# Seven block products for w_in as well, in pair sets, and block sums by adding transfers

## The reference

```python
h = x @ w_in;  r = np.maximum(h, 0.0);  g = r * r;  x = g @ w_out      # first MLP
h = x @ w_in;  g = h * (1.0 / (1.0 + np.exp(-h)));  out = g @ w_out     # second MLP
```

## Time and profile before

| | before |
|---|---|
| median of 3 runs | 532.4 us (532.11 to 532.63) |
| profiled execution | 531.69 us, span 529.9 us |
| granted TensorE clock, mean | 0.999 |
| PE busy | 521.0 us (98%), 2628 instructions |
| DVE busy | 350.9 us (66%) |
| ACT busy | 260.3 us (49%) |
| POOL busy | 77.5 us (15%), all before 95 us |
| DMA | 42.17 MB |

### The profile page before, as it was taken

The page is one execution under the profiler, slowest core; times in us unless marked ns, Lnnn a source line. Parts: engine busy times, 40 slices in busy tenths (PEclk is TensorE's granted clock), DMA queues, the critical chain, the costliest instruction groups (busy, mean ns, idle before and its releaser), DMA issues.

```text
span 529.9 us, 7052 instructions
## 1 busy us (share of the span) xinstructions
PE 521.0 (98%) x2628; PEld 440.0 (83%) x2628; DVE 350.9 (66%) x604; ACT 260.3 (49%) x404; POOL 77.5 (15%) x52
## 2 busy tenths in 40 slices
PE   7999999999999999999999999999999999999996
PEld 5333335799999999999999999999999999999996
DVE  3487878797687533667799746556764245568975
ACT  5999996154454333544444344454444144454220
POOL 1899999000000000000000000000000000000000
PEclk9999999999999999999999999999999999999999
DMA  7798611051302202522032025202211241020447
GB/s 222 196 241 227 180 41 33 28 141 59 80 0 80 59 1 59 141 59 67 13 80 61 1 61 139 61 18 62 60 49 32 61 138 36 26 80 10 102 74 106
DMA packets 82181, 42.17 MB, mean 80 GB/s; under 512 B 26848, under 2 KB 79072, under 8 KB 82144
## 3 DMA queue, kind: packets, MB, share of 16 engines
q1 hardware_dynamic: 77984, 40.32, 29.2%
q10 hardware_dynamic: 4128, 1.38, 1.1%
q0 software_dynamic: 32, 0.00, 0.0%
HBM read 38.93 MB, written 2.75 MB: 79 GB/s over the span
## 4 chain that ended last, share of the span: by engine, by line
PE 94%; DMA 2%; DVE 1%; ACT 1%; issue 1%; SPq 1%; ACTq 0%
PE banks L558 27%; PE banks L557 27%; PE banks L559 27%; PE banks L477 4%; PE banks L470 4%; PE banks L498 2%; PE banks L467 1%; DMA qk_raw<-in_k_dram 1%; DMA qk_raw<-in_q_dram 1%; PE banks L489 1%; ACT prob L683 1%; SPq L324 1%; ACT prob L690 0%; DVE asum L917 0%; ACTq L660 0%
## 5 line engine op out<-in xcount | busy, mean ns | idle before, releaser
L557 PE MATMUL banks<-x_hi,w_hl 128*128 128x448 f32 x384 | 139.4, 363 | 0.0
L558 PE MATMUL banks<-x_lo,w_hl 128*128 128x448 f32 x384 | 139.4, 363 | 0.0
L559 PE MATMUL banks<-x_hi,w_hl 128*128 128x448 f32 x384 | 138.3, 360 | 0.0
L558 PE MATMUL banks<-g_lo,w_hl 128*128 128x448 f32 (+1 forms) x340 | 122.7, 361 | 0.0
L557 PE MATMUL banks<-g_hi,w_hl 128*128 128x448 f32 (+1 forms) x340 | 122.5, 360 | 0.0
L559 PE MATMUL banks<-g_hi,w_hl 128*128 128x448 f32 (+1 forms) x340 | 121.7, 358 | 0.0
L557 PEld LDWEIGHTS banks<-x_hi,w_hl 128*128 128x128 f32 x384 | 72.1, 188 | 6.9 <-issue 1.4
L559 PEld LDWEIGHTS banks<-x_hi,w_hl 128*128 128x128 f32 x384 | 71.8, 187 | 5.1
L558 PEld LDWEIGHTS banks<-x_lo,w_hl 128*128 128x128 f32 x384 | 72.1, 188 | 3.8
L975 DVE TENSOR_TENSOR w_hl<-w_raw,w_hl 128x768 fp32r<-128x768 f32 x32 | 31.9, 996 | 55.4 <-ACT w_hl L716 55.2
L557 PEld LDWEIGHTS banks<-g_hi,w_hl 128*128 128x128 f32 x340 | 63.8, 188 | 4.8
(11 more groups left out here) (63 smaller groups left out, 509.8 us busy)
## 6 DMA issues: line engine op xcount, KB each, us to landing
w_raw<-in_moe_w_in_dram SPq DMA_DIRECT2D x32, 384.0 KB, 3.4
w_raw<-in_moe_w_out_dram SPq DMA_DIRECT2D x24, 512.0 KB, 5.2
qk_raw<-in_k_dram SPq DMA_DIRECT2D x44, 112.0 KB, 2.7
qk_raw<-in_q_dram SPq DMA_DIRECT2D x44, 112.0 KB, 3.3
v_t<-in_v_dram SPq DMA_DIRECT2D x24, 96.0 KB, 2.8
out_dram<-rows SPq DMA_DIRECT2D x38, 56.0 KB, 2.2
qk_raw<-in_k_dram ACTq DMA_DIRECT2D x4, 112.0 KB, 3.0
qk_raw<-in_q_dram ACTq DMA_DIRECT2D x4, 112.0 KB, 4.0
```

The source lines that it names most:

```text
L557: pe.matmul(dst, hi[:, kk, :], mov_hi, start=start, stop=False, skip_group_check=onto)
L558: pe.matmul(dst, hi[:, kk, :], mov_lo, start=False, stop=False, skip_group_check=onto)
L559: return pe.matmul(dst, lo[:, kk, :], mov_hi, start=False, stop=stop, skip_group_check=onto)
```

## The change

- w_in is computed with seven block products too, in all stages but the first. A *pair set* makes two hidden chunks by two batches: 7 products of 3 x 3 passes. x therefore needs seven operands (`x_all`, B11 to T4, high and low), of which four are sums (`xt_make`).
- A layer has three stages of 2, 3 and 3 chunk pairs instead of two of 8 chunks. The order of sets in a layer is: the stage's pair sets, then its three group sets. The very first stage has two *plain sets* (72 passes each) in place of pair sets, and x's sums are made beside them. All sets are numbered in `sets`; 0 and 1 are plain.
- Signs are arranged so that a block sum of weights is an addition. The four sums of a set (q1 to q4, one product each: 1, 4, 2, 5) are no longer made by DVE but by DMA transfers that add onto their destination, issued by GpSimd (q1 from DRAM, the others from SBUF). The blocks that are added to are loaded once more for it: six loads of one block each and four adding transfers per set.
- In a pair set ACT copies the results of products 0 to 2 into `work`, DVE adds products 3 to 5 onto them, ACT applies relu or silu (`shape`, for C11, C22, C12 after takes 3, 4, 5 and for C21 from the bank after product 6), and ACT squares (`square`), where DVE did before.
- `w_hl` has 4 slots of one block instead of 3; PSUM banks alternate between sets (0 to 3 and 4 to 7).
- In attention the sums of denominators are transposed straight from PSUM, the small constant is added to 14 columns afterwards, `add_last_rest` moves ahead of the inversion of the last pair but one, and `split` writes a third product, x unsplit, into y's space.

```diff
-    STAGES = 2
+    KP = KC // 2
+    SIZES = (2, 3, 3)
+    BEGIN = (0, 4, 10)
+    STAGES = len(SIZES)
...
+            def add_q3(s):
+                pool.wait_ge(s_raw[s.no % 2][0], loads_of(s))
+                pool.wait_ge(s_raw[s.no % 2][2], loads_of(s))
+                add_weights(raw_block(s, 1, 0), raw_block(s, 0, 0)).then_inc(s_q3, DMA)
+            def add_q4(s):
+                pool.wait_ge(s_raw[s.no % 2][1], loads_of(s))
+                pool.wait_ge(s_w_lo, s.first + 3)
+                add_weights(q_block(s, 1), raw_block(s, 0, 1)).then_inc(s_q4, DMA)
...
+            for s, ahead in zip(sevens[1:], sevens):
+                add_q1(s)
+                add_q3(s)
+                add_q4(ahead)
+                add_q2(s)
...
+            def bank_taken(s, n):
+                of = {2: 0, 4: 2, 5: 1, 6: 4}[n]
+                if of in copied_by_scalar(s):
+                    pe.wait_ge(s_copy, copy_no[s.no, of])
                 else:
+                    pe.wait_ge(s_take, take_no[s.no, of])
+            def operands(s, n, kk):
+                if s.kind == GROUP and s.i == 0:
+                    pair = sets[s.no - 1]
+                    if n == 0 and kk == 0:
+                        pe.wait_ge(s_g, NP * pair.pair)
+                    if kk == s.k - 1:
+                        pe.wait_ge(s_g, g_no(pair, n))
...
+            def prod_high(s, n):
                 if n in (0, 3, 6):
+                    act.wait_ge(s_raw[s.no % 2][{0: 0, 3: 1, 6: 3}[n]], loads_of(s))
                 else:
+                    act.wait_ge({1: s_q1, 2: s_q2, 4: s_q3, 5: s_q4}[n], DMA * (s.seven + 1))
+                act.wait_ge(s_prod, s.first + n + 1 - SLOTS)
+                act.activation(prod_split(s, n)[0], prod_source(s, n), ACT.Copy).then_inc(s_w_hi, 1)
+            def copy(s, n):
+                act.wait_ge(s_prod, s.first + n + 1)
+                if s.kind == PAIR:
+                    work_free(act, s, AFTER[n])
...
```

DVE's order, from the diff. `take(s, n)` adds a bank onto y or work; a group set takes all seven (in stages 1 and 2), a pair set 3 to 5:

```diff
+            x_sums(0)
+            plain_low(two, 0)
+            t_make(one, N_T1)
+            g_low(one, N_B11)
+            g_low(one, N_T1)
+            x_operands(0)
+            x_sums(1)
+            plain_low(two, 1)
...
+            x_operands(1)
+            x_sums(2)
+            x_operands(2)
+            prod_low(sets[2], 0)
+            t_make(two, N_T1)
+            g_low(two, N_B11)
+            g_low(two, N_T1)
+            prod_low(sets[2], 1)
+            for s in sets[2:]:
+                ahead = sets[s.no - 1]
+                after = sets[s.no + 1] if s is not LAST else None
+                for n in range(NP):
+                    if n == 0 and 6 in taken_by_vector(ahead):
+                        take(ahead, 6)
+                    if n > 0 and n - 1 in taken_by_vector(s):
+                        take(s, n - 1)
+                    if n + 2 < NP:
+                        prod_low(s, n + 2)
+                    elif after:
+                        prod_low(after, n + 2 - NP)
+                    if s.kind == PAIR and n == 5:
+                        g_low(s, N_B11)
+                    if s.kind == PAIR and n == 6:
+                        g_low(s, N_B22)
+                    if ahead.kind == PAIR:
+                        if n == 0:
+                            t_make(ahead, N_T1)
+                            g_low(ahead, N_T1)
+                            t_make(ahead, N_T2)
+                            t_make(ahead, N_T3)
+                        if n == 1:
+                            g_low(ahead, N_T2)
+                            g_low(ahead, N_T3)
+                        if n == 2:
+                            g_low(ahead, N_B21)
+                            t_make(ahead, N_T4)
+                        if n == 3:
+                            g_low(ahead, N_T4)
...
+                    if makes_x(ahead):
+                        if n == 0:
+                            xt_make(1, ahead.i, N_T3)
+                            xt_make(1, ahead.i, N_T1)
+                        if n == 1:
+                            x_low(1, ahead.i, N_T1)
+                            xt_make(1, ahead.i, N_T2)
...
```

More of the change, by code:

```diff
@@ L15 @@
 DMA = 16
+PLAIN, PAIR, GROUP = range(3)
+@dataclass(frozen=True)
+class Set:
+    no: int
+    layer: int
+    stage: int
+    kind: int
+    i: int
+    k: int
+    first: int
+    pair: int
+    seven: int
 def attention_then_two_mlps(nc, q, k, v, cap, w_in1, w_out1, w_in2, w_out2, out):
@@ new lines, in x_source, with x_group, makes_x, leaves @@
+        def x_source(kk, n):
+            block = {N_B11: C11, N_T1: C12, N_T2: C11, N_B21: C21, N_T3: C22, N_B22: C22, N_T4: C21}[n]
+            return y_tile(*out_tile(kk, block))
+        def x_group(kk):
+            return [s for s in sets if makes_x(s) and s.i == kk][0]
+        def makes_x(s):
+            return s.layer == 0 and s.stage == STAGES - 1 and s.kind == GROUP
+        def leaves(s):
+            return s.layer == 1 and s.stage == STAGES - 1 and s.kind == GROUP
+        def work_free(eng, s, block):
+            if s.pair == 0:
+                return
+            ahead = [o for o in sets if o.kind != GROUP and o.pair == s.pair - 1][0]
+            users = {C11: (N_B11, N_T1), C12: (N_T1, N_T3), C22: (N_B22, N_T2, N_T3), C21: (N_B21, N_T4)}[block]
+            eng.wait_ge(s_g, max(g_no(ahead, n) for n in users))
@@ new lines, in hidden_plain, with banks_free @@
+            def hidden_plain(s, r):
+                pe.wait_ge(s_w_lo, s.first + 2 * r + 2)
+                for c in range(2):
+                    for kk in range(KP):
+                        for b in range(B):
+                            last = passes(bank(s, 2 * r + b), prod_split(s, 2 * r + c), kk, x_of(PLAIN_X[b][c], kk),
+                                          c + kk == 0, c == 1 and kk == KP - 1)
+                    last.then_inc(s_prod, 1)
+            def banks_free(s):
+                ahead = sets[s.no - 2]
+                if taken_by_vector(ahead):
+                    pe.wait_ge(s_take, take_no[ahead.no, taken_by_vector(ahead)[-1]])
+                if ahead.kind == GROUP and ahead.stage == 0:
+                    pe.wait_ge(s_copy, copy_no[ahead.no, 6])
+                if ahead.kind != GROUP:
+                    pe.wait_ge(s_relu if ahead.layer == 0 else s_z, 4 * (ahead.pair + 1))
@@ new lines, in product @@
+            def product(s, n):
+                pe.wait_ge(s_w_lo, s.first + n + 1)
+                if n == 0:
+                    banks_free(s)
+                parted = s is LAST and n == NP - 1
+                onto = n in ONTO and not parted
+                if onto:
+                    bank_taken(s, n)
+                for part, cols in enumerate(LAST_COLS if parted else (slice(0, S),)):
+                    dst = last_bank(part) if parted else bank(s, BANK_OF[n])
+                    for kk in range(s.k):
+                        operands(s, n, kk)
+                        mov = x_of(n, kk) if s.kind == PAIR else (g_tile(n, kk, 0), g_tile(n, kk, 1))
+                        last = passes(dst[:, cols], prod_split(s, n), kk, [a[:, cols] for a in mov],
+                                      kk == 0 and not onto, kk == s.k - 1, onto)
+                    last.then_inc(s_prod, 1)
@@ new lines, in x_high @@
+            def x_high(layer, kk, n):
+                if n in (N_B11, N_B21, N_B22):
+                    act.wait_ge(s_take, take_no[x_group(kk).no, {N_B11: 3, N_B22: 4, N_B21: 6}[n]])
+                else:
+                    act.wait_ge(s_xt, xt_no(layer, kk, n))
+                    if layer == 0 and n == N_T1:
+                        act.wait_ge(s_prod, sets[2].first)
+                act.activation(x_tile(n, kk, 0), x_source(kk, n), ACT.Copy).then_inc(s_xo_hi, 1)
+            one, two = sets[0], sets[1]
@@ new lines, in _ @@
+            for block in (C11, C12):
+                shape(one, block)
+            plain_high(two, 0)
+            for block in (C11, C12):
+                square(one, block)
+            g_high(one, N_B11)
+            g_high(one, N_T1)
+            for n in (N_T2, N_T3, N_T4):
+                x_high(0, 0, n)
+            for block in (C22, C21):
+                shape(one, block)
+            plain_high(two, 1)
+            for block in (C22, C21):
+                square(one, block)
+            for n in (N_T2, N_B21, N_T3, N_B22, N_T4):
+                g_high(one, n)
```

1002 lines of the change are left out of this document (486 added, 516 removed).

## The result

After the change the median is 555.5 us (555.35 to 556.84, 4 runs); before, on the same chip, 532.5 (532.11 to 532.8, 4 runs). The ratio is 1.0438 [1.0426, 1.0451]. The prediction said 540.0 in a range of 525 to 558, slower with 0.73: direction and range held, the size did not (+7.6 forecast, +23.0 measured).

What follows compares the result with a forecast made beforehand. PE's issued passes were taken to set the time, as long as DVE and ACT keep up: 531.69 - 25.2 - 0.5 + 17.0 + 3.7 + 3.3 + 8.2 + 1.1 = 539.3 profiled, plus 0.7 gives 540.0 us, range 525 to 558.

Steps and rivals of the forecast that it cites:

- What PE loses (-25.2): PE's w_in passes fall from 1152 to 1026; 126 fewer at 0.200 us save 25.2 us.
- Attention (-0.5): In attention add_last_rest moves ahead of the inversion, so PE's 0.55 us wait before its last sums goes: -0.5 us.
- The start (8.2): Layer 0's first stage: DVE's list makes PE late at product 0 and until take 4 at 137.5: 8.2 us.
- The turns of a pair set: DVE-ACT turns make a pair set's loop 13.3 us against PE's 12.6; four stages of three pairs lose 17.0 us.
- The adding transfers at 0: The weight sums by DMA land in 3.9 us, in time for prod_high 5, and cost PE nothing.
- Rival (b): The adding transfers land late, at 5.2 us, moving the loop 1.3 us in 15 sets: 20 us more, 560; chance 0.15.
- x's operands (3.3): Layer 0 stage 2: group sets making x's seven operands lose 2.1 us, then layer 1's product 1 waits 1.2.
- Layer 1, stage 0 (3.7): Two pair sets lose 0.5 us, then short group-set products find g_low T1, T2, B21 and take 4 late: 3.7.
- Restarts (1.1): After a wait PE's second pass starts 0.31 us after the first instead of 0.20; about ten uncovered stalls: 1.1 us.

Runs made afterwards that it cites:

- e1: The changed kernel without its adding transfers, so the weight sums are missing: 549.99 us, 1.0336 to the kernel before.
- e2: The changed kernel with x's third tile (sums and operands) moved from ahead of the first group set into the second: 552.04 us, 1.0368 to the kernel before.
- e3: The changed kernel with ACT writing g_hi B11 and B22 ahead of the next shape in pair sets: 546.5 us, 1.0272 to the kernel before.
- e5: On e2 and e3 together (541.15 us): g_low B22 between t_make T1 and its g_low, g_hi T1 before the square of C21: 538.67 us.
- e15: The changed kernel with only prod_high 5, which waits for q4, one product later in all sets, behind the copies: 550.77 us, 1.0345 to before.
- e8: The changed kernel without storing products C11 and C22 of the last set: 555.06 us, 1.0415 to the kernel before.
- e9: On e5 plus an earlier take 0 (537.2 us): stage 0's group sets do copies 1 and 2 before prod_high 5: 536.46 us.
- e10: On e9: T3 and T1 of the next x made at the end of their own set, the others one product earlier: 535.38 us.
- e11: On e10: t_make T4 one product later in group sets, behind take 2: 534.65 us, 1.0046 to the kernel before.

## Why the prediction was right in direction and short in size

The step that failed is the one on the adding transfers, put at 0 where e1 puts 5.5 us on them. The tail, also at nothing, cost 2.6, and the terms for the turns and for x's operands were too small by 3.8 and 2.0 us.

- **What PE loses (-25.2): right.** 1026 passes, and wherever nothing holds PE they start 0.200 us apart as in the earlier trace rows.
- **Attention (-0.5): wrong.** The wait of 0.55 before PE's last sums did go (they start at 96.01 with no idle time), but PE came to this place 0.9 later: the first MLP pass starts at 88.14 us, 87.23 before. The last pass of the plain sets starts at 122.03, 121.75 before: +0.3.
- **The start (8.2): right in place, and in size almost.** Product 0 at 124.86 (124.5 predicted), take 4 freeing PE at 138.24 (137.5); 8.9 in all, the low clock inside it. e2 showed that x's third tile was the cause of the first stall, and that moving it leaves half of the stage's excess in waits behind it.
- **The turns of a pair set: the mechanism right, the size 3.8 too small.** The loop of 13.6 against 13.3 and the 0.65 us of idle time per turn stand in the rows; e3 and e5 remove turns and the time goes, 9.0 and 2.5 us. Without adding transfers (e1) the four stages have 20.8 us of excess, 17.0 predicted. Layer 1's two stages came to 4.7 and 5.7 (0.8 of it low clock) against 3.8 each. In layer 0 (6.4 and 5.6 against 4.7 each) the size was off: ACT's list with the squares is full there, as e3's timeline shows, and the prediction gave it 0.3 a set.
- **The adding transfers at 0: the step that failed.** The time to land was right (3.6 to 3.8, taken as 3.9), but "ACT wants it for prod_high 5 at about 4.1 to 4.4, so it has 3.9 us" compared it with prod_high 5 alone, in a set that runs steadily, and at 4.1 it has 3.55 only. ACT waited for q4 16 times, up to 3.4 us, in stages of every kind. At nine of these places PE's excess is the same without adding transfers (e1). In the short group sets of stage 0, in the pair set behind them and in the sets that make x, what PE needs stands behind that wait in ACT's list, and there PE waited. e1 puts 5.5 us on it (0.9 of that is the low clock at 510), e15 4.8 for the order alone. Rival (b) named this wait and priced it at 20, as if every set's loop moved; it was a quarter of that.
- **x's operands (3.3): 6.2, or 5.3 without adding transfers.** The group sets were nearly right (1.7 against 2.1). The first pair set of layer 1 was not: I let one product wait for the last x; three did (326.69, 329.36, 332.42), each for its own x_low, then one more at 337.57. 4.5 instead of 1.2.
- **Layer 1, stage 0 (3.7): 5.0, and 1.6 at 380.56,** which is the q4 wait again.
- **Restarts (1.1): too small, but not measured by itself.** Each start after a wait costs 0.15 before the first pass and about 0.1 at the second (400.99, 401.14, 401.42), at some 35 places. Where DVE's loop is the bound this is covered, so how much of the excess it is stays open.
- **The clock: a missing term,** about 0.8 us in the profiled execution (at 510), and it varies between executions, 0.7 to 2.2 us a stretch (e8, e2).
- **The tail: a missing term, 2.6 us.** It is shorter by 1.5 without two stores, so stores are part of it. In e8 the DMA share is 0.55 from 548 to 554, and the tail is still 5.6 where before's is 4.5; what this rest is stays open. That the DMA engines are full in after's tail is shown by its windows (columns as above):

```profile
546.00:552.00 6.00, 0.25 (x3) 0.08 (x1) 1.32 (x4) 0.00 (x0) 0.00 (x0) 0.94 1.02 142
```

In sum, with e1's trace to tell the terms apart: 5.5 us the adding transfers, 3.8 the turns of the four stages, 2.0 x's operands, 1.4 layer 1's stage 0, 0.7 the start, less the 1.1 for restarts, which are in these rows already; 2.6 for the tail and 0.8 for attention. That is 15.7, where 15.5 are to be explained.

## What to carry to other kernels

Before work is taken from the busiest engine, write out the orders of the engines that feed it: at 66% and 49% busy neither could follow a PE with 126 passes less, since one chained round trip between them costs 1.25 us and holds all that is queued behind it. Price a transfer not by when its reader wants it but by what is queued behind the reader's wait, at the seams of stages too, and put what the bounding engine needs ahead of that wait (4.8 us by moving one instruction of each set). Expect a mended stall to come back in part at the next instruction of the list: of the gains expected for e2, e9, e10 and e11 a fifth to a half was kept.

## What was not expected of the hardware

- An adding transfer of 192 KB took 3.6 to 3.8 us from issue to landing within SBUF and 6.1 with a DRAM source, where SP's plain loads of the same size from DRAM took 2.5 to 3.9; its issue kept GpSimd for 0.84 and 1.61 us.
- The granted clock fell to 0.50 in a wait of 2.47 us in after, and at the same place in e1 only in the wait behind it (2.45 us, three passes, 1.50 us). After two waits of 0.98 and 0.99 us it fell in one execution and not in another, and after 0.55 and 1.00 us it fell as well.
- The stores at the end move 142 GB/s with a DMA share of 1.02 in the window 546 to 552 above: the DMA engines' time was full at that rate. In the page of after (DMA share in tenths and GB/s by slice) the third and fourth slice moved 238 and 239 GB/s at 9 tenths:

```profile
DMA  7799702224878676877666663579877677776677
GB/s 230 192 238 239 212 7 66 50 49 80 185 160 169 138 146 125 166 162 148 139 136 138 146 127 62 100 159 192 156 145 147 130 158 156 147 146 143 120 103 101
```
